# The low parts of a two-layer MLP's weights, made on GpSimd in pieces of 256 columns in place of 768 and 1024

## The reference, cut to what matters

```python
def _moe_ref(x, w_in, w_out):            # layer 1: 512 -> 2048 -> 512
    h = x @ w_in
    g = h * (1.0 / (1.0 + np.exp(-1.702 * h)))
    return (g @ w_out).astype(np.float32)

def _moe2_ref(x, w_in, w_out):           # layer 2, same shapes
    h = x @ w_in
    g = np.maximum(h, 0.0) + np.log1p(np.exp(-np.abs(h)))
    return (g @ w_out).astype(np.float32)
```

## Time and profile before

| | us |
|---|---|
| three runs | 1023.02, 1026.78, 1027.03 |
| their median | 1026.78 |
| the profiled execution | 1023.06 |
| its span (first to last instruction) | 1021.3 |
| PE busy (matmuls) | 868.1 (85%) |
| DVE busy | 698.9 (68%) |
| POOL busy | 540.9 (53%) |
| ACT busy | 433.8 (42%) |
| mean granted TensorE clock | 0.931 of full |

### The profile page before, as it was taken

One profiled execution on the slowest core, in us unless ns is written; L12 is line 12 of the kernel. 1 busy time (PEld: TensorE's weight loads), 2 busy tenths in 40 slices (PEclk: granted clock), 3 DMA queues, 4 the chain that ended last, 5 costly groups with the idle time before them and its releaser, 6 DMA issues.

```text
span 1021.3 us, 12292 instructions
## 1 busy us (share of the span) xinstructions
PE 868.1 (85%) x4584; PEld 774.1 (76%) x4584; DVE 698.9 (68%) x1029; ACT 433.8 (42%) x751; POOL 540.9 (53%) x416
## 2 busy tenths in 40 slices
PE   7857999789999899997788888668888866888797
PEld 6747888779999788887677776557776755877686
DVE  4666565884555965758767777767777776777753
ACT  4532323342223333233554455454545455454443
POOL 1675656634444436565566665445666544665531
PEclk9978999989999999999989998888999888899999
DMA  9812121010101011211110010002001001200001
GB/s 317 305 42 78 47 78 47 21 41 22 42 21 42 22 59 45 83 42 42 46 58 21 22 42 21 22 22 82 22 22 42 21 21 33 72 21 22 22 1 62
DMA packets 22219, 53.28 MB, mean 52 GB/s; under 512 B 2064, under 2 KB 7824, under 8 KB 22160
## 3 DMA queue, kind: packets, MB, share of 16 engines
q1 hardware_dynamic: 21584, 52.17, 15.2%
q10 hardware_dynamic: 576, 0.33, 0.1%
HBM read 47.78 MB, written 4.72 MB: 51 GB/s over the span
## 4 chain that ended last, share of the span: by engine, by line
DVE 36%; PE 35%; ACT 10%; POOL 8%; issue 7%; DMA 3%; DVEq 0%; POOLq 0%; ACTq 0%
PE ps L514 19%; DVE gs_f L879 9%; PE ps L553 8%; POOL fix L378 8%; DVE gs_f L848 5%; PE ps L556 4%; ACT gs L675 4%; DVE gs L883 4%; DVE xs L812 3%; DVE xs_f L801 3%; DVE gs_f L856 3%; PE ps L559 3%; DVE fix L867 3%; DVE gs_f L875 2%; DMA kv_in_sb<-k_v 2%
## 5 line engine op out<-in xcount | busy, mean ns | idle before, releaser
L514 PE MATMUL ps<-xs,w_in 128*128 128x384 f32 x2016 | 443.1, 363 | 126.1 <-DVE gs_f L848 111.8
L514 PEld LDWEIGHTS ps<-xs,w_in 128*128 128x128 f32 x2016 | 380.8, 205 | 161.3 <-issue 101.5
L357 POOL TENSOR_TENSOR w_in<-w_in_f,w_in 128x1024 fp32r<-128x1024 f32 x96 | 217.2, 2268 | 75.4 <-ACT w_in L680 75.2
L559 PE MATMUL ps<-w_out,gs 128*128 128x512 f32 x864 | 234.0, 409 | 9.0 <-DVE gs L883 8.7
L378 POOL TENSOR_TENSOR fix<-ex,fix 128x384 f32<-128x384 f32 x96 | 111.5, 1161 | 216.8 <-DVE fix L867 216.8
L553 PE MATMUL ps<-gs,w_out 128*128 128x512 f32 x576 | 209.1, 396 | 0.0
L559 PEld LDWEIGHTS ps<-w_out,gs 128*128 128x128 f32 x864 | 168.4, 199 | 43.8 <-issue 16.0
L848 DVE TENSOR_TENSOR gs_f<-ps,gs_f 128x384 f32<-128x384 f32 x240 | 130.8, 550 | 90.6 <-PE ps L514 89.1
L556 PE MATMUL ps<-gs,w_out 128*128 128x256 f32 x576 | 162.8, 283 | 0.0
L879 DVE TENSOR_TENSOR gs_f<-gs_f,fix 128x384 f32<-128x384 f32 x96 | 96.5, 1005 | 61.8 <-POOL fix L378 61.1
L883 DVE TENSOR_TENSOR gs<-gs_f,gs 128x384 fp32r<-128x384 f32 x96 | 91.2, 950 | 52.4 <-ACT gs L675 50.1
(11 more groups left out here) (58 smaller groups left out, 728.3 us busy)
## 6 DMA issues: line engine op xcount, KB each, us to landing
w_in_f<-w_in SPq DMA_DIRECT2D x48, 512.0 KB, 3.3
kv_in_sb<-k_v SPq DMA_DIRECT2D x16, 512.0 KB, 8.7
w_out_f<-w_out SPq DMA_DIRECT2D x16, 512.0 KB, 4.1
q_sb<-q_t SPq DMA_DIRECT2D x16, 288.0 KB, 9.4
out<-xy SPq DMA_DIRECT2D x18, 256.0 KB, 3.8
tail_sb<-k_v SPq DMA_DIRECT2D x3, 256.0 KB, 11.8
tail_sb<-k_v ACTq DMA_DIRECT2D x1, 256.0 KB, 5.0
eye_sb<-eye ACTq DMA_DIRECT2D x1, 64.0 KB, 5.6
```

The lines of the kernel that those rows point to most:

```text
L357: nc.gpsimd.tensor_tensor(w[:, LO, slots], w_in32[:, n % W_BUFS, LO, slots], w[:, HI, slots].bitcast(F32), ALU.subtract).then_inc(w_split, 1)
L514: mm = nc.tensor.matmul(ps[:, bank, 0:HALF], w[:, wp, W_OF[k], cols], xs[:, k, xp, t], start=(new and t == 0 and (wp, xp) == (HI, HI)), st ...
L559: mm = nc.tensor.matmul(ps[:, ACC_BANK + j, 0:DM], g[:, j * P:(j + 1) * P], w, start=new, stop=done)
```

## The change

`w_low` gets a list of slots in place of a slice and issues one subtraction of 256 columns for each slot; slots 0 to 3 and 4 to 6 are now named by W_OF, the order in which the products use them. `w_out_low` issues four subtractions of 256 columns in place of one of 1024. Each increments its semaphore, so the counts that TensorE waits for are 7 for a step's w_in and 4 for a pair of w_out, where they were 2 and 1. What is computed, the places of the groups in GpSimd's order, and all other engines' orders are as before. In all 96 + 16 instructions become 336 + 64.

```diff
             def w_low(n, slots):
-                w = w_in[:, n % W_BUFS]
-                nc.gpsimd.tensor_tensor(w[:, LO, slots], w_in32[:, n % W_BUFS, LO, slots], w[:, HI, slots].bitcast(F32),
-                                        ALU.subtract).then_inc(w_split, 1)
+                w, w32 = w_in[:, n % W_BUFS], w_in32[:, n % W_BUFS]
+                for slot in slots:
+                    nc.gpsimd.tensor_tensor(w[:, LO, slot], w32[:, LO, slot], w[:, HI, slot].bitcast(F32),
+                                            ALU.subtract).then_inc(w_split, 1)
...
             def w_out_low(m):
                 pair, layer = w_out_of(m)
-                w = w_out[:, 2 * pair:2 * pair + 2]
                 pool.wait_ge(w_out_hi, STEPS * layer + pair + 1)
-                nc.gpsimd.tensor_tensor(w[:, :, LO], w_out32[:, 2 * pair:2 * pair + 2, LO], w[:, :, HI].bitcast(F32),
-                                        ALU.subtract).then_inc(w_out_split, 1)
+                for f in (2 * pair, 2 * pair + 1):
+                    for cols in (slice(0, DM // 2), slice(DM // 2, DM)):
+                        nc.gpsimd.tensor_tensor(w_out[:, f, LO, cols], w_out32[:, f, LO, cols],
+                                                w_out[:, f, HI, cols].bitcast(F32), ALU.subtract
+                                                ).then_inc(w_out_split, 1)
...
-                    w_low(n, slice(0, 4))
+                    w_low(n, W_OF[0:4])
...
-                    pe.wait_ge(w_split, 2 * m + 2)
+                    pe.wait_ge(w_split, 7 * (m + 1))
...
-                        pe.wait_ge(w_out_split, phase * STEPS + p + 1)
+                        pe.wait_ge(w_out_split, 4 * (phase * STEPS + p + 1))
```

More of the change, by code:

```diff
@@ L364, in w_all @@
                 pool.wait_ge(w_hi_early, n + 1)
-                w_low(n, slice(0, 4))
-                w_low(n, slice(4, 7))
+                w_low(n, W_OF[0:4])
+                w_low(n, W_OF[4:7])
             def w_out_low(m):
                 pair, layer = w_out_of(m)
-                w = w_out[:, 2 * pair:2 * pair + 2]
                 pool.wait_ge(w_out_hi, STEPS * layer + pair + 1)
-                nc.gpsimd.tensor_tensor(w[:, :, LO], w_out32[:, 2 * pair:2 * pair + 2, LO], w[:, :, HI].bitcast(F32),
-                                        ALU.subtract).then_inc(w_out_split, 1)
+                for f in (2 * pair, 2 * pair + 1):
[3 more added lines that the diff above has]
+                                                ).then_inc(w_out_split, 1)
             def softplus_fix(m, tile):
```

## The result

| | before | changed |
|---|---|---|
| median, us | 1024.9 (4 runs) | 990.13 (4 runs) |
| lowest to highest | 1022.09 to 1027.03 | 987.94 to 991.23 |
| profiled execution, its span | 1023.06, 1021.3 | 987.94, 986.1 |
| mean granted TensorE clock | 0.931 | 0.962 |

The ratio is 0.966, 95% interval 0.9626 to 0.9693: the changed kernel takes 34.8 us less. The forecast was 986. One execution further down, the profiled one of the kernel with pieces of 64 columns, fell in the chip's slower state; its steps and single rows are read, its total is not compared.

The account below looks back on a forecast made before the run. No engine is full; DVE's two-SBUF-input operations wait for GpSimd's long subtractions. Terms 23.2 + 7.8 + 2.4 - 0.2 - 2.2 + 7.5 = 38.5 us off 1023.06 give 984.6, stated as 986; range 968 to 1006.

Parts of the forecast that it names:

- Turns eat more: Rival, chance 0.12: more pieces meet waiting DVE operations; plain steps win 0.8 us, w_out steps lose 0.45; 1007 us.
- VectorE wins the ties: Rival, chance 0.15: line 883 goes ahead of pieces 2 and 7 in layer 2's plain steps, winning 34 us; 974 us.
- No hand-over inside a group: Rival, chance 0.07: GpSimd keeps the ports from piece to piece, so DVE waits for whole groups; 30 us slower, 1053 us.
- the order is strict turns: At the SBUF ports DVE and GpSimd share: who waits while the other holds goes next; a turn costs DVE 0.43 us.
- Nothing happens: Rival, chance 0.05: another wait of the same length replaces the one removed, likely PE's products in layer 2; 1023 us.
- Plain steps of layer 2: Layer 2 steps without chunk end or w_out work: 20.38 to 18.93 us, 16 x 1.45 = 23.2 us won.
- Chunk ends in layer 2: Steps 31, 32, 39, 40: line 801 waits for one piece, not the long instruction; 7.8 us won in all.
- Step 24: Line 812 behind w_out's low part wins 1.9 us and its 879 wins 0.5: 2.4 us won.
- Step 25: Eleven pieces make the fix of C21 slip by 0.7 us, spending what 879 wins: -0.2 us.
- Steps of layer 1 with w_out work: Steps 1 to 6, 18 to 22: four turns, 1.77 us, replace a 1.6 us wait; 0.2 lost each, 2.2 in all.
- Steps 10 to 14: Layer 1 steps without w_out work: 856 ends at 273.90 in place of 273.93, so no change, 0 us.
- Chunk ends of layer 1 and step 0: Steps 7, 8, 15, 16, 23 and step 0: DVE waits less behind long low parts; 7.5 us won in all.

Follow-up runs that it names:

- the kernel with long pieces and w_out early: The kernel before, subtractions uncut, with w_out's low part in layer 1 moved directly behind the sums: 1039.66 us, ratio 1.0146.
- the uneven cut: The changed kernel with w_in's pieces of 288, 256, 256, 224 and 256, 288, 224 columns in place of even 256: 975.4 us, ratio 0.9521.

## Why the prediction was right, point by point

**The mechanism.** DVE stands behind GpSimd for the rest of one instruction and is let in at its end. This was borne out in 882 (0.98 against a forecast 1.0), in 886 (1.12 against 1.14), and by the two ties that went to GpSimd as in the earlier trace rows. *Turns eat more* fell by the plain steps and by those with w_out work: 1.50 won and 0.20 lost, where it wanted 0.8 and 0.45. The rival *VectorE wins the ties* fell by the rows of 886 after. The kernel that makes it come true has 975.4 where the rival said 974, but this agreement is in part luck: that rival put a plain step at 18.2 with PE as its bound, where 17.96 was measured, and the steps with w_out work lost 0.44 in place of 0.2. *No hand-over inside a group* fell by 882 alone: 0.98 with 2.74 us of pieces over it. It fell for pieces of 256 columns; with 64 it comes true in layer 1. So "the order is strict turns" holds for this change and is no general rule. *Nothing happens* fell by the total.

**Plain steps of layer 2**, forecast 23.2: measured 23.5. Fourteen of them won 1.50, steps 26 and 41 won 1.30 and 1.20.

**Chunk ends in layer 2**, forecast 1.8 each in 31 and 39 and 2.1 each in 32 and 40: measured 1.80 and 1.84, but 0.44 and 1.57. Step 24, forecast 2.4: 0.91. Step 25, forecast -0.2: -0.14.

**Steps of layer 1 with w_out work**, forecast -0.2 each, -2.2 in all: measured -0.18 to -0.23 in ten of them, +0.31 in step 1, -1.7 in all. The turns are there as laid out. In step 3 (timeline, DVE) four operations of the gate in a row are held, and a fifth is not:

```profile
126.08 0.78 DVE L862 CAST gs<-gs_f 128x384 fp32r<-128x384 f32 x1
126.89 0.97 DVE L864 TENSOR_TENSOR gs<-gs_f,gs 128x384 fp32r<-128x384 f32 x1
127.79 1.09 DVE L859 TENSOR_TENSOR gs_f<-gs_f,lg 128x384 f32<-128x384 f32 x1
128.91 0.78 DVE L862 CAST gs<-gs_f 128x384 fp32r<-128x384 f32 x1
129.73 0.56 DVE L864 TENSOR_TENSOR gs<-gs_f,gs 128x384 fp32r<-128x384 f32 x1
```

With 0.56 for 864, 0.55 for 859 and 0.36 for 862 alone that is 0.42 + 0.41 + 0.54 + 0.42 = 1.79 us of waiting, where I had 1.77. Steps 10 to 14 were forecast at 0 and are 15.60 on both sides.

**Chunk ends of layer 1 and step 0**, forecast 7.5. Here lies the step that was mis-sized: 7 and 23 won 1.26 each (forecast 1.6), step 15 1.18 (0.5), step 0 4.39 (2.4), and steps 8 and 16, forecast to win 0.7 each, lost 0.82 and 0.90. For the losses the granted clock is the likely reason. Columns: the stretch, its length, busy time of PE, PEld, DVE, ACT and POOL, then the granted clock, DMA share and GB/s. Before, around the border of steps 7 and 8 (P1 of 8 at 209.63):

```profile
204.00:209.60 5.60, 5.45 (x16) 4.60 (x17) 5.28 (x11) 2.34 (x5) 0.00 (x0) 0.51 0.29 94
209.60:228.83 19.23, 16.23 (x92) 14.69 (x91) 16.57 (x22) 8.84 (x15) 8.87 (x6) 1.00 0.05 10
```

After, with P1 of step 8 at 204.53:

```profile
204.50:206.60 2.10, 2.07 (x7) 2.10 (x8) 2.07 (x3) 0.44 (x1) 2.10 (x2) 0.50 0.00 0
206.60:208.00 1.40, 1.40 (x6) 1.21 (x5) 1.09 (x2) 0.48 (x1) 0.31 (x1) 0.57 0.00 0
208.00:224.40 16.40, 14.19 (x81) 12.68 (x79) 11.00 (x18) 7.87 (x13) 6.36 (x7) 1.00 0.04 10
```

And PE's rows there, before and after:

```profile
204.15 2.29 PE L514 MATMUL ps<-xs,w_in 128*128 128x384 f32 x6 [4.57 <-DVE gs_f L848]
```

```profile
204.53 2.26 PE L517 MATMUL ps<-xs,w_in 128*128 128x384 f32 x6 [5.48 <-DVE gs_f L851]
```

Before, PE idled for 4.57 us ahead of the last product of step 7 and then ran at the lower level (1.2 GHz) to the end of that step; step 8 had the full 2.4 GHz throughout. After, the wait inside step 7 is gone, PE idles for 5.48 us ahead of P1 of step 8, and 3.5 us at the lower level fall into step 8. The two steps together went from 42.26 to 41.82 us: as I read it, step 7's gain was in part a slow stretch handed on to step 8. Step 16 shows the same (mean clock 1.00 before, 0.91 after), step 24 too (0.93 and 0.87). Step 32 got 0.81 and took 27.15, step 40 got 0.91 and took 25.98 with the same instructions. Step 0 went the other way, 0.76 to 0.92: the 12 matmuls that took 3.63 us before take 2.34, which may be 1.3 us of the 2.0 it won above the forecast. In steps 9 and 17, identical in work, 15.68 and 17.25 us change places between kernels as the clock is 1.00 or 0.90. My sum had no term for the clock. Against the forecast, steps 0 and 15 brought 2.7 us more and 7, 8, 16, 23, 24, 32 and 40 brought 7.5 us less; of the steps named, the clock differs as told in 0, 8, 16, 24 and 32.

Is the clock behind the gain of the plain steps too? Their mean granted clock rose from 0.92 to 1.00. No: in the kernel with long pieces and w_out early, plain steps 26 to 28 had the full clock and took as long as before. Step 26, in the columns from above:

```profile
543.83:564.19 20.36, 16.18 (x78) 13.94 (x79) 15.30 (x22) 10.18 (x19) 12.51 (x10) 1.00 0.08 27
```

And step 33 of the changed kernel, at 0.91, took 18.87. Steps 26 and 41, at 0.91 and 0.85, took 19.07 and 19.15, which may be the part of their gain that is missing.

In sum the span fell by 35.2 us where 38.5 were forecast. With 987.94 the profiled execution stands 3.3 us above the forecast 984.6, and the median 4.1 above 986.

What stays open: why the clock falls in one step and not in its twin was not settled; that it falls behind a long idle stretch of PE is seen at the border of steps 7 and 8, and not tested by a run of its own. Nor was it followed up why step 15 won twice its forecast, or why a VectorE operation misses its turns in 19 steps with 64-column pieces.

## What to carry to other kernels

Where GpSimd and VectorE read SBUF on the same path, the length of GpSimd's instruction is what VectorE may have to wait, and cutting it can pay even when it makes GpSimd's total longer, as long as the row of pieces ends before GpSimd's next urgent work. Measure more than one size, since at 64 columns one VectorE operation in each of 19 steps stood through many pieces. Do not stop at an even cut: read from the timeline at what distance the waiting instruction comes, and place the end of the piece so that it falls behind its arrival and the next piece does not start ahead of it. In a plain step 32 columns in the right place were worth twice what halving all pieces was (0.90 and 0.46 us); in the total halving was worth more (965.4 against 975.4), since the uneven cut did nothing for the chunk ends and lost in the steps with w_out work. When work is moved, lay out the whole row at its new place, and where a wait of TensorE goes, look for where its idle time will lie next, since the matmuls behind a long one may run at half the clock.

## What the runs showed of the hardware

**A turn has a price on both sides, and the fixed part of a GpSimd subtraction is large.** From piece to piece, undisturbed: 256 columns 0.70 us, 128 columns 0.43 (3.40 for eight). Halving the columns saves 0.27 us and not 0.35, so about 0.15 us of each piece doesn't shrink. 64 columns are 0.28 us apart. Over a whole run, turns with DVE included, w_in's pieces of 256, 128 and 64 columns keep GpSimd busy for 286.2 us (336 of them), 356.4 (672) and 471.5 (1344).

**A tie of 0.02 us is stable.** The plain steps from 27 on repeat within 0.02 us, but for the first behind a chunk end: 18.85 to 18.87 in the changed kernel, where GpSimd wins both ties, and 17.95 to 17.97 with the uneven cut, where DVE is 0.05 us ahead. That so small a distance decides the same way in every step was not in the forecast, which gave the other side a chance of 0.15.

**Not every wait ends with a piece.** With pieces of 128 columns and more a held VectorE operation got in after at most two of them. With 64 columns one gate multiply in each of 19 steps stood still while 7 to 13 whole pieces passed (up to 4.25 us).

**A cast is held as well.** The gate's high part, a cast with one input in SBUF, takes 0.78 us beside a piece in place of 0.36, while the add that reads PSUM keeps its 0.55.

**The clock falls for single stretches within a step.** It was at 0.50 to 0.57 for 5.6 us behind PE's idle 4.57 us, and for 3.5 us behind its idle 5.48 us, and 1.00 right after. Where that stretch lies is worth 1 to 2 us of a step of 16 to 20.
